# One routing table through DRAM once instead of twice, and the search passes of two routing rounds at other steps

## The reference

```python
# attention: q, k, v of (4, 12, 448, 64)
scores = scale * np.matmul(q, k.transpose(0, 1, 3, 2)) - np.log(S)
attn = 1.0 / (1.0 + np.exp(-scores))
x = np.matmul(attn, v)              # then turned to (1792, 768)

# routed experts: N = 1792 tokens, E = 8 experts, each takes cap = 224
order = np.argsort(-(x @ w_gate).flatten())
for idx in order:                   # the best (token, expert) pair first
    tok, e = idx // E, idx % E
    if assigned[tok] >= 0 or counts[e] >= cap: continue
    assigned[tok] = e; counts[e] += 1
for e in range(E):
    mask = assigned == e
    out[mask] = np.maximum(x[mask] @ w1[e], 0.0) @ w2[e]   # w1 768x1024

# dense layer: w_in 768x2048, w_out 2048x768
h = x @ w_in
out = (np.maximum(h, 0) + alpha * np.minimum(h, 0)) @ w_out
```

## Time and profile before

| | before |
|---|---|
| time of the runs, median | 1022.49 us |
| time of the profiled execution | 1022.49 us |
| its span | 1020.6 us |
| PE busy | 994.8 us (97%) |
| DVE busy | 573.3 us (56%) |
| ACT, POOL busy | 389.6, 185.1 us |
| DMA | 222.38 MB, mean 218 GB/s |

### The profile page before, as it was taken

One profiled execution on the slowest core, in us unless ns is written; L12 is line 12 of the kernel. 1 busy time (PEld: TensorE's weight loads), 2 busy tenths in 40 slices (PEclk: granted clock), 3 DMA queues, 4 the chain that ended last, 5 costly groups with the idle time before them and its releaser, 6 DMA issues.

```text
span 1020.6 us, 16700 instructions
## 1 busy us (share of the span) xinstructions
PE 994.8 (97%) x6533; PEld 857.3 (84%) x6533; DVE 573.3 (56%) x1299; ACT 389.6 (38%) x625; POOL 185.1 (18%) x200
## 2 busy tenths in 40 slices
PE   8999999998999999899999999999999999999997
PEld 5555555567999999899999999999999999999996
DVE  4444444598668637958952775596448537221212
ACT  5776767401151123356122225641122356121212
POOL 0101100106240001244201024340100425200001
PEclk9999999997999999999999999999999999999999
DMA  9999997407389686666978746579695435976601
GB/s 208 277 276 264 274 265 237 169 10 258 101 292 372 217 214 216 253 161 216 326 282 214 257 164 159 176 237 365 228 248 196 144 132 183 347 276 218 214 14 54
DMA packets 123139, 222.38 MB, mean 218 GB/s; under 512 B 53104, under 2 KB 70896, under 8 KB 123072
## 3 DMA queue, kind: packets, MB, share of 16 engines
q1 hardware_dynamic: 89120, 121.14, 38.0%
q0 software_dynamic: 20976, 90.61, 28.2%
q10 hardware_dynamic: 12976, 9.70, 3.9%
HBM read 184.84 MB, written 36.58 MB: 217 GB/s over the span
## 4 chain that ended last, share of the span: by engine, by line
PE 90%; DVE 6%; ACT 1%; issue 1%; DMA 1%; POOLq 0%; POOL 0%; DVEq 0%; ACTq 0%
PE psum L973 23%; PE psum L987 21%; PE psum L920 11%; PE psum L950 10%; PE psum L712 8%; PE psum L696 7%; DVE hits L1564 3%; PE psum L915 2%; PE psum L680 2%; PE psum L723 1%; PE psum L945 1%; DMA stage<-x_rows,tok_idx 1%; PE psum L867 1%; PE psum L731 1%; PE psum L855 1%
## 5 line engine op out<-in xcount | busy, mean ns | idle before, releaser
L973 PE MATMUL psum<-y_high,unit 128*128 128x448 f32 x768 | 229.6, 368 | 0.5 <-DVE y_low L1478 0.4
L987 PE MATMUL psum<-g_high,unit 128*128 128x448 f32 x756 | 226.8, 368 | 0.9 <-DVE g_low L1489 0.9
L973 PEld LDWEIGHTS psum<-y_high,unit 128*128 128x128 f32 x768 | 144.3, 188 | 12.4 <-issue 1.2
L987 PEld LDWEIGHTS psum<-g_high,unit 128*128 128x128 f32 x756 | 142.0, 188 | 12.6 <-DVE g_low L1489 1.6
L973 PE MATMUL psum<-y_low,unit 128*128 128x448 f32 x384 | 140.2, 365 | 0.0
L987 PE MATMUL psum<-g_low,unit 128*128 128x448 f32 x378 | 138.1, 365 | 0.0
L1461 DVE TENSOR_TENSOR unit<-raw,unit 128x768 fp32r<-128x768 f32 (+1 forms) x106 | 109.7, 1059 | 38.9 <-ACT unit L1145 28.7
L1171 ACT ACTIVATE above<-psum 128x448 f32<-128x448 f32 x64 | 34.9, 546 | 245.9 <-PE psum L973 245.9
L1484 DVE SCALAR_TENSOR_TENSOR below<-below,neg_alpha,above 128x448 f32<-128x448 f32 x64 | 43.8, 684 | 146.9 <-ACT below L1172 144.7
L920 PE MATMUL psum<-x_high,unit 128*128 128x224 f32 x672 | 117.7, 276 | 0.0
L950 PE MATMUL psum<-h_high,unit 128*128 128x224 f32 x672 | 115.7, 276 | 1.4 <-issue 1.4
(11 more groups left out here) (184 smaller groups left out, 1321.5 us busy)
## 6 DMA issues: line engine op xcount, KB each, us to landing
unit<-ffn_parts SPq DMA_DIRECT2D x120, 768.0 KB, 6.7
ffn_parts<-pre_parts POOLq DMA_DIRECT2D x24, 768.0 KB, 6.2
ffn_parts<-unit SPq DMA_DIRECT2D x8, 768.0 KB, 6.8
q_in<-in_q_dram SPq DMA_DIRECT2D x24, 224.0 KB, 5.3
v_in<-in_v_dram SPq DMA_DIRECT2D x24, 224.0 KB, 7.4
x_rows<-x_tok POOLq DMA_DIRECT2D x8, 672.0 KB, 5.7
k_in<-in_k_dram SPq DMA_DIRECT2D x23, 224.0 KB, 6.9
pre_raw<-in_moe_w_in_dram ACTq DMA_DIRECT2D x12, 384.0 KB, 7.9
```

Source lines behind the costliest of these rows:

```text
L973: last = pe.matmul(psum[:, in_bank(m), 0:PAIR], w, y[:, c, :], start=(c == 0 and i == 0), stop=(c == DC - 1 and i == 2))
L987: last = pe.matmul(psum[:, OUT_BANK + d, 0:PAIR], w, g[:, m % 2, :], start=(m == 0 and i == 0), stop=(m == (FC - 1 if q < GROUPS - 1 else ...
```

## The change

The tensor `third_flat` is gone. For round 2 SP stores `suit` once into `suit_flat[0]` (8 rows) and loads `rank_in` from it with the access pattern that POOL uses for the later rounds: 8 rows, each repeated 16 times. The semaphore waits follow. In the tables of rounds 2 and 3 most passes and the three later parts stand one or two steps earlier; the steps of the transposes of the gathered tokens (41 and on, `STEPS + 5` and on) are the same.

```diff
-    third_flat = nc.dram_tensor("third_flat", (2 * E, P * G), F32).ap()
                 if r == 2:
-                    passes, later = (21, 22, 23, 24, 28, 30, 31, 32), (34, 35, 37, 41)
+                    passes, later = (21, 22, 23, 24, 25, 28, 30, 31), (33, 34, 36, 41)
                 elif r == 3:
-                    passes, later = (43, 45, 47, 48, 50, 51, 53, 54), (55, 57, 59, STEPS + 5)
+                    passes, later = (42, 43, 44, 46, 48, 50, 51, 52), (54, 56, 58, STEPS + 5)
...
             sp.wait_ge(suit_done, 3)
-            for half in range(2):
-                sp.dma_start(third_flat.rearrange("(e h) (p g) -> h p e g", h=2, g=G)[half], suit[:]
-                             ).then_inc(third_stored, 16)
-            sp.wait_ge(third_stored, 32)
+            sp.dma_start(suit_flat[0].rearrange("e (p g) -> p e g", g=G), suit[:]).then_inc(third_stored, 16)
+            sp.wait_ge(third_stored, 16)
             sp.wait_ge(*loaded(w2_unit(1, EC - 3)))
-            sp.dma_start(rank_in[:], third_flat.unsqueeze(1).to_broadcast([2 * E, DIGIT // 2, P * G])
-                         ).then_inc(third_loaded, 16)
+            sp.dma_start(rank_in[:], suit_flat[0].unsqueeze(1).to_broadcast([E, DIGIT, P * G])).then_inc(third_loaded, 16)
```

## The result

The changed kernel takes 1031.97 us (median of 8 runs, 1030.22 to 1036.31), the kernel before on the same chip 1023.93 us (8 runs, 1021.64 to 1027.12). The ratio is 1.0075, 95% interval 1.0052 to 1.0096: slower by 0.75%, 8 us. I had forecast 1026.4 us and a range up to 1031.0.

A forecast was written before the change was run, and what follows sets the result against it. PE was taken to bound the kernel (busy 994.8 of 1020.6 us), so only its waits counted. Terms of +2.86, +1.6, +1.7, -2.3 and 0 summed to +3.9 us on 1022.5: 1026.4 us, range 1021.0 to 1031.0.

The forecast's parts named there:

- the two places that I named: PE's 2.6 us wait for round 3's `thr_rows` at step 54, and step 28, without slack behind `y_low`.
- Term 1: Round 2, step 28: a fifth pass ahead of `y_low` makes PE start later, +2.86 us.
- Term 2: Round 2's `rank_in` load lands after DVE wants it, delaying passes, `y_low` and PE: +1.6 us, between 0 and 5.6.
- The bounds that I gave: Round 2's load, issue to landing: 7.9 us (same queue, other source) to 16.2 us (same source, POOL's queue).
- Term 3: PE's idle gap at step 28 makes the granted clock fall once, +1.7 us.
- The 3.4 us that I had priced for a longer gap: Clock loss after PE stands some 8.9 us at step 28, in the case of the slowest load.
- Term 4: Round 3, step 54: the `thr_rows` wait goes, a little returns at `g_low`; -2.3 us.
- Term 5: One store instead of two on SP's queue: any gain ahead of 306 us is lost again, 0 us.
- the load is the bound: Rival: round 2's load as slow as POOL's slower one, first pass waits 5.6 us; +9.6 us, 1032.0 us, chance 0.17.
- the clock holding: Part of a rival at step 28: load in time, clock does not fall; +0.3 us, 1022.8 us, chance 0.27.

The follow-up runs named there:

- e1: Kernel before with the new tables of rounds 2 and 3 but the old store and 16-row load; ratio 1.0025, 1027.10 us.
- p2: Changed kernel with SP waiting for round 2's load to land before its next issue; trace only, landing after 11.4 us.
- e5: Kernel before with only round 3's new table; ratio 0.9992, 1022.18 us.
- e3: Changed kernel with round 2's load split into eight DMAs, one per expert, each one row read 16 times; ratio 1.0032, 1027.72 us.
- e4: e1 with the load split into two DMAs of 64 partitions, each with a leading dimension of 8; ratio 1.0049, 1030.14 us.
- p3: e3 with SP waiting for round 2's load to land before its next issue; trace only, landing 8.2 us after first issue.
- p4: e4 with SP waiting for round 2's load to land before its next issue; trace only, landing 10.2 us after first issue.
- e6: Kernel before with only round 2's new table, old store and load; ratio 1.0051, 1029.26 us.
- e7: Kernel before with round 3's passes at 43, 44, 46, 47, 48, 50, 51, 52, later parts from step 54; ratio 0.9970, 1020.34 us.
- e8: e3 with the old table of round 2 and e7's table of round 3; ratio 0.9974 against the kernel before, 1021.04 us.
- p1: Kernel before with SP waiting for round 2's load to land before its next issue; trace only, landing after 8.4 us.
- e2: Changed kernel with the old tables of rounds 2 and 3, keeping the new store and 8-row load; ratio 1.0039, 1028.05 us.

## Why the prediction was wrong

**Where PE waits and what the change touches.** Right for the two places that I named. I missed a third, the `x_low` of step 44, and the `g_low` of step 59. From the start of the second duo to the end the two traces agree within 0.1 us (577.3 and 577.4 us).

**Term 1, the fifth pass ahead of `y_low`, +2.86 us.** Right: 2.88 us in e1, 2.87 us for the pass in the changed kernel.

**Term 2, the load, +1.6 us.** This is the step that failed most, by its size. The mechanism was as told: narrow load, first pass, five passes, `y_low`, PE. But I took 12.2 us for the load, the quieter of POOL's two, and it took 15.0; DVE waited 4.8 us for it instead of 1.6. The 12.2 was too small for two reasons. First, I priced the traffic behind the load on SP's own queue at nothing; with it held back (p2) the load took 11.4 us, with the traffic running 15.0. Second, it was short even for POOL's load: I read it off the packets of the queue, and the landing comes after them: in e5 the last small packets lie in 374 to 375 us and DVE's wait for the load ends at 375.37, 13.8 us after its issue at 361.62. In the five profiles whose view of the DMA issues gives POOL's loads a landing time, the median is 13.7 to 15.0 us. The rest of the difference, 0.4 us, is the cover: from SP's issue to the time at which DVE was ready lay 10.6 us before (295.40 to 306.00) and 10.2 us after (293.34 to 303.53). Both moved about 2 us ahead in this execution, so the earlier reader by itself cost next to nothing. The bounds that I gave, 7.9 and 16.2 us, did hold the load.

**Term 3, the clock, +1.7 us.** The low stretch came, at step 28, in the profiles of the changed kernel, e1, e3, e4, p2, p3 and p4, and stayed away in e6. In the changed kernel it cost about 1.4 us, since it lay mostly in the idle time. The 3.4 us that I had priced for a longer gap was too much here for that reason. In e4 the low stretch (0.53 in 320 to 330 us) reached about 5 us past the gap of 6.7 us, whose end was at 325.44: at half the clock an estimated 2.6 us of loss.

**Term 4, round 3's table, -2.3 us.** Half right, and the second step that failed. The wait for `thr_rows` went, and the threshold was in time as worked out. I did not look at the other end of the table: at step 42 the first pass is ahead of POOL's load, and the rows on POOL's load were in my hands. That cost 1.5 us between the starts of steps 43 and 44, and another 0.9 us went at the end, most of it for a `g_low`. So the term was about 0 in the profile instead of -2.3; e5 shows 0.8 us of gain, with an interval that holds 0. e7 is this term with that mistake undone.

**Term 5, the single store, 0.** No run isolates it. e3 and e8, with one store, lie beside e1 and e7, with two, within their intervals.

**The rivals and the range.** The rival "the load is the bound" was the right one, with 1032.0 us for a measured 1031.97. Its parts were partly lucky: load and clock were both priced higher than they came (5.6 for 4.8, 3.4 for 1.4 us), and round 3's gain at 2.3 us for about 0. Two prices too high and one gain too large cancelled out. I gave it 0.17 although both of my rows for loads of this shape, on POOL's queue, lay at 12 us and above, and I let the range end at 1031.0, below that case. The probability and the range were too kind to the taken value: the case that hangs on the one unknown cost should have been inside. What spoke for the clock holding, that a gap of 2.55 us had left it alone, rested on one execution; in three of four profiles such a gap did not.

## What to carry to other kernels

Look at the leading dimension of a load whose source is a few rows, each repeated. Here 8 instead of 16 cost 3 us by itself (11.4 against 8.4 us) and 6 to 7 us with other loads behind it (15.0 against 7.9 to 9.2), and eight small DMAs of 16 partitions each did as well as a second copy in DRAM. Before an instruction is moved ahead in a hand-written order, look at both sides: what it waits for at the new place (round 3's first pass came ahead of its load), and what stands behind it on its engine (`y_low`, `x_low`). Where a term hangs on a transfer that has to land before its reader is ready, take the landing and not the last packets, and take the cover from several executions: from SP's issue to DVE's readiness it lay between 9.5 us (p4) and 13.9 us (e6, which had a low clock ahead of it) in these profiles.

## What the runs showed of the hardware

A load with a leading dimension of 8 was slowed by loads issued behind it on the same queue (11.4 us without them, 15.0 with them), while one with a leading dimension of 16 was not, as far as the executions tell (8.4 and 7.9 to 9.2 us).

In e4 the gather of a unit of weights, on POOL's queue, made ACT wait 3.4 us and DVE 3.3 us at the same time. It is not shown that the narrow load did this: in the changed kernel, with a narrow load and the same traffic behind it, ACT's waits for gathers at that time are 1.1 us in all, the longest 0.5.

A gap of 2.5 us in PE's matmuls was followed by a granted clock of 1.00 in one execution (the kernel before), and of 0.57 over 4 us, 0.72 over 6 us and 0.53 over 7 us in three others (p1, e2, e6). After the gaps of 3.3 us and more at step 28 (the changed kernel, e1, e3, e4, p2, p3, p4) the profiles show a low stretch each time, except in e6, where the gap was 3.3 us and the clock stayed at 1.00.
